# Agent attention with a two-layer feed-forward: the linear part's left-over rows on two row groups, a different last sum, and eight key slots

## What is computed

```python
def sm(a, b):
    s = scale * (a @ b.transpose(0, 2, 1))
    s = s - s.max(-1, keepdims=True)
    e = np.exp(s)
    return e / (e.sum(-1, keepdims=True) + 1e-09)
agent_v = sm(agents, k) @ v
x = (sm(q, agents) @ agent_v).reshape(B * N, C)
h = x @ w_in
g = np.maximum(h, 0.0) + alpha * np.minimum(h, 0.0)
out = g @ w_out
```

## Time and profile before

| | |
|---|---|
| median of 3 runs | 918.34 us (917.63 to 918.72) |
| profiled execution, its own time | 918.38 us |
| its span | 916.5 us |
| TensorE (PE) busy | 907.9 us, 99% |
| VectorE (DVE) busy | 626.0 us, 68% |
| ScalarE (ACT) busy | 514.8 us, 56% |
| GpSimd (POOL) busy | 108.4 us, 12% |
| mean DMA traffic | 72 GB/s, 298 and 336 GB/s in the first two fortieths |

### The profile page before, as it was taken

One profiled execution on the slowest core, in us unless ns is written; L12 is line 12 of the kernel. 1 busy time (PEld: TensorE's weight loads), 2 busy tenths in 40 slices (PEclk: granted clock), 3 DMA queues, 4 the chain that ended last, 5 costly groups with the idle time before them and its releaser, 6 DMA issues.

```text
span 916.5 us, 16103 instructions
## 1 busy us (share of the span) xinstructions
PE 907.9 (99%) x5662; PEld 488.7 (53%) x5662; DVE 626.0 (68%) x923; ACT 514.8 (56%) x695; POOL 108.4 (12%) x138
## 2 busy tenths in 40 slices
PE   9999999999999999999999999999999999999998
PEld 9865555555555565555444444444444444444443
DVE  4567667677777777677776666767676766767664
ACT  2445555555555555656565655555565656566554
POOL 6500010010010010010010101001010101010101
PEclk9999999999999999999999999999999999999999
DMA  8952222221232233121121111111111212111100
GB/s 298 336 164 87 60 72 88 60 82 54 73 96 97 72 92 100 38 57 35 38 58 34 43 52 40 54 38 56 37 57 37 57 36 59 34 49 44 33 29 22
DMA packets 67813, 65.75 MB, mean 72 GB/s; under 512 B 38528, under 2 KB 63424, under 8 KB 67520
## 3 DMA queue, kind: packets, MB, share of 16 engines
q1 hardware_dynamic: 67488, 65.19, 23.8%
q10 hardware_dynamic: 288, 0.06, 0.0%
HBM read 40.49 MB, written 12.78 MB: 58 GB/s over the span
## 4 chain that ended last, share of the span: by engine, by line
PE 95%; DMA 2%; issue 2%; DVE 1%; SPq 0%; ACT 0%; POOLq 0%
PE ps L599 56%; PE ps L582 18%; PE ps L589 7%; PE ps L563 3%; PE ps L609 2%; PE ps L772 2%; PE ps L766 1%; PE ps L519 1%; PE ps L441 1%; DMA kv_s<-kT 1%; DMA w_inT_s<-w_inT 1%; PE ps L544 1%; DVE r_lo L1181 0%; PE ps L465 0%; PE ps L472 0%
## 5 line engine op out<-in xcount | busy, mean ns | idle before, releaser
L1181 DVE SCALAR_TENSOR_TENSOR r_lo<-ps,r_hi 128x960 f16<-128x960 f32 x416 | 466.5, 1153 | 248.0 <-ACT r_hi L938 245.6
L938 ACT ACTIVATE r_hi<-ps 128x960 f16<-128x960 f32 x416 | 386.2, 967 | 173.9 <-PE ps L589 173.8
L599 PE MATMUL ps<-r_hi,w_hi 128*128 128x480 f16 x832 | 252.1, 369 | 0.5 <-DVE r_lo L1181 0.5
L599 PE MATMUL ps<-r_hi,w_lo 128*128 128x480 f16 x832 | 248.0, 366 | 0.0
L599 PE MATMUL ps<-r_lo,w_hi 128*128 128x480 f16 x832 | 240.8, 366 | 0.0
L582 PE MATMUL ps<-PT,M_a 128*128 128x480 f16 x832 | 203.2, 366 | 0.3 <-DVE r_lo L1181 0.3
L426 POOL TENSOR_TENSOR y<-y_relu,y_lin 128x480 f32<-128x480 f32 x52 | 62.3, 1199 | 616.0 <-ACT y_relu L1019 443.6
L599 PEld LDWEIGHTS ps<-r_hi,w_lo 128*128 128x128 f16 x832 | 91.2, 110 | 68.8
L582 PEld LDWEIGHTS ps<-PT,M_a 128*128 128x128 f16 x832 | 81.1, 99 | 86.3 <-DVE r_lo L1181 2.1
L599 PEld LDWEIGHTS ps<-r_lo,w_hi 128*128 128x128 f16 x832 | 85.4, 106 | 71.2
L599 PEld LDWEIGHTS ps<-r_hi,w_hi 128*128 128x128 f16 x832 | 73.2, 106 | 81.5 <-issue 38.8
(11 more groups left out here) (153 smaller groups left out, 515.5 us busy)
## 6 DMA issues: line engine op xcount, KB each, us to landing
q_s<-qT SPq DMA_DIRECT2D x52, 240.0 KB, 2.6
out<-y SPq DMA_DIRECT2D x52, 240.0 KB, 2.0
kv_s<-kT SPq DMA_DIRECT2D x23, 512.0 KB, 4.3
kv_s<-vP SPq DMA_DIRECT2D x12, 512.0 KB, 9.5
kv_s<-vS SPq DMA_DIRECT2D x8, 768.0 KB, 4.4
PR<-PT SPq DMA_DIRECT2D x156, 32.0 KB, 1.8
PT<-stack SPq DMA_TRANSPOSE x208, 2.3
w_lin<-w_out SPq DMA_DIRECT2D x1, 1024.0 KB, 8.5
```

The source lines that it names most:

```text
L599: mm = pe.matmul(ps[:, OUT, 0:CHUNK], w[:, 2 * p + u, :], r[:, s, u, :], start=(p == 0 and u == 0 and k == 0), stop=(p == PAIRS - 1 and u ...
L938: act.activation(r_hi[:, p % RING, :, :], ps[:, at:at + 2, 0:CHUNK], ACT.Relu).then_inc(hi_ready, 1)
L1181: dve.scalar_tensor_tensor(out=r_lo[:, p % RING, :, :], in0=ps[:, at:at + 2, 0:CHUNK], scalar=0.0, in1=r_hi[:, p % RING, :, :], op0=ALU.ma ...
```

## The change

- linear: L_a as two matmuls of 240 columns into banks 0 and 1; the 32 rows that L_b really has come later, behind rest_of_quad(3), as two matmuls of 240 columns, one on row group 0 (PT) and one on row group 1 (PR). L_b has 64 rows, the 32 twice, and GpSimd no longer clears it. mix_linear writes the 32 rows to partitions 0 to 31 and 32 to 63.
- ScalarE takes y_lin after relu_hi of pair 6 instead of before it, from two banks. SyncE's turn waits for lin_ready instead of h_ready.
- The last chunk has no y_relu and no sum on GpSimd: VectorE adds bank 6, scaled, and y_lin in two halves of 240 columns; SyncE stores the first, ScalarE's queue the second.
- Keys go through all 8 slots, w_out is loaded behind piece 6, the values' first load waits until piece 8 has been scored; the clearing of slots 4 to 7 to ones stands behind piece 8, the maximum of w_relu behind piece 9, and relu_max_row behind piece 12. 5 and 3 matmuls on ones instead of 6 and 4.

```diff
+HALF = CHUNK // 2
+KEY_SLOTS = 2 * RING
...
-        L_b = sb("L_b", [128, B, C], F16)
-        L_rh = sb("L_rh", [32, C], F16)
+        L_b = sb("L_b", [64, B, C], F16)
+        L_rh = sb("L_rh", [64, C], F16)
...
             def load_keys(m):
-                s = (m - 1) % RING
-                if m > RING:
+                s = (m - 1) % KEY_SLOTS
+                if m > KEY_SLOTS:
 
-                    sp.wait_ge(k_scored, m - RING + 1)
+                    sp.wait_ge(k_scored, m - KEY_SLOTS + 1)
...
             def load_values(m):
+                if m == 1:
+
+                    sp.wait_ge(k_scored, KEY_SLOTS + 1)
...
                 load_keys(m)
-                if m == 3:
+                if m == 6:
                     sp.dma_start(w_lin[:, :, :], w_out).then_inc(in_wo, 16)
...
-                    sp.wait_ge(h_ready, groups)
+                    sp.wait_ge(lin_ready, parts)
...
-                    sp.wait_ge(y_ready, n + 1)
-                    sp.dma_start(out[n], y[:, half, :]).then_inc(stored[half], 16)
+                    if there(n + 1):
+
+                        sp.wait_ge(y_ready, n + 1)
+                        sp.dma_start(out[n], y[:, half, :]).then_inc(stored[half], 16)
+                    else:
+
+                        sp.wait_ge(last_y, 1)
+                        sp.dma_start(out[n][:, 0:HALF], y[:, half, 0:HALF]).then_inc(stored[half], 16)
...
-            pool.memset(L_b[:, :, :], 0.0).then_inc(consts, 1)
...
-                    finish(n, half, i)
+                    if there(n + 1):
+                        finish(n, half, i)
...
             def mix_linear(b, bank):
                 pe.wait_ge(b_avl, b + 1)
-                pe.matmul(ps[0:32, bank, C:2 * C], av_l[:, b, 128:SEL], lin_w[:, :], start=True, stop=True,
-                          skip_group_check=True)
+                for g in (0, 32):
+                    pe.matmul(ps[g:g + 32, bank, C:2 * C], av_l[:, b, 128:SEL], lin_w[:, :], start=True, stop=True,
+                              skip_group_check=True)
...
             def linear(half, b):
-                for w, end in ((L_a, False), (L_b, True)):
-                    mm = pe.matmul(by_tile(ps[:, 2 * LIN_SLOT, 0:CHUNK]), w[:, b, :], tokens(PT, half), start=not end,
-                                   stop=end)
+                for h in range(2):
+                    pe.matmul(by_tile(ps[:, 2 * LIN_SLOT + h, 0:HALF]), L_a[:, b, :], tokens(PT, half)[:, 2 * h:2 * h + 2, :],
+                              start=True, stop=False)
+
+
+            def rest_of_linear(half, b):
+                for h, src in enumerate((PT, PR)):
+                    at = slice(32 * h, 32 * h + 32)
+                    mm = pe.matmul(by_tile(ps[:, 2 * LIN_SLOT + h, 0:HALF]), L_b[at, b, :],
+                                   tokens(src[at, :, :], half)[:, 2 * h:2 * h + 2, :], start=False, stop=True)
                 mm.then_inc(lin_ready, 1)
...
-            warm(6)
+            warm(5)
             pe.wait_ge(in_agents, 16)
             tail_scores(0, SMALL)
-            warm(4)
+            warm(3)
             for m in range(1, FULL + 1):
                 first_scores(m)
-                if m == FULL - 1:
-
-                    pe.wait_ge(consts, 5)
-                    relu_max_row()
+
+            pe.wait_ge(consts, 4)
+            relu_max_row()
...
                     rest_of_quad(3, half, b)
+                    rest_of_linear(half, b)
                     second_layer(4, half)
...
+                    relu_hi(g + 6, quad + 3, 6, False)
                     act.wait_ge(lin_ready, n + 1)
                     if not (isinstance(i, int) and i == 0):
 
                         act.wait_ge(y_ready, n - 1)
-                    act.activation(y_lin[:, half, :], ps[:, 2 * LIN_SLOT, 0:CHUNK], ACT.Copy,
+                    act.activation(y_lin[:, half, :].rearrange("p (h n) -> p h n", n=HALF),
+                                   ps[:, 2 * LIN_SLOT:2 * LIN_SLOT + 2, 0:HALF], ACT.Copy,
                                    scale=lin_unscale[:, b, :]).then_inc(lin_saved, 1)
-                    relu_hi(g + 6, quad + 3, 6, False)
...
+                    else:
+
+                        act.wait_ge(last_y, 2)
+                        act.dma_start(out[n][:, HALF:CHUNK], y[:, half, HALF:CHUNK]).then_inc(stored[1 - half], 16)
...
-                if m == 7:
+                if m == 9:
                     dve.wait_ge(relu_w_in, 1)
                     dve.tensor_reduce(w_col[:, 0:1], w_relu[:, :, :], AX.XY, ALU.max,
                                       apply_absolute_value=True).then_inc(relu_col, 1)
-                if m == FULL - 1:
-                    relu_max_top()
+                if m == KEY_SLOTS:
+
+                    for s in range(RING, KEY_SLOTS):
+                        dve.memset(kv_s[:, s, 0:4 * RUN + 1:RUN], 1.0).then_inc(ones_in, 1)
             key_max_column(0)
+            relu_max_top()
...
+                    else:
+
+                        dve.wait_ge(lin_saved, n + 1)
+                        dve.wait_ge(pair_done, g + PAIRS)
+
+                        dve.wait_ge(stored[half], 16 * i)
+                        for at in (slice(0, HALF), slice(HALF, CHUNK)):
+                            dve.scalar_tensor_tensor(out=y[:, half, at], in0=ps[:, OUT, at], scalar=out_unscale[:, b, :],
+                                                     in1=y_lin[:, half, at], op0=ALU.mult, op1=ALU.add).then_inc(last_y, 1)
```

More of the change, by code:

```diff
@@ L152, in build @@
         in_agents, in_acol, in_wo, in_wT = sem("in_agents"), sem("in_acol"), sem("in_wo"), sem("in_wT")
-        in_k = [sem(f"in_k{s}") for s in range(RING)]
+        in_k = [sem(f"in_k{s}") for s in range(KEY_SLOTS)]
         in_v = [sem(f"in_v{s}") for s in range(2 * RING)]
@@ L184, in build @@
         h_ready, hi_ready, lo_ready, pair_done = sem("h_ready"), sem("hi_ready"), sem("lo_ready"), sem("pair_done")
-        lin_ready, lin_saved, relu_saved, y_ready = (
-            sem(x) for x in ("lin_ready", "lin_saved", "relu_saved", "y_ready"))
+        lin_ready, lin_saved, relu_saved, y_ready, last_y = (
+            sem(x) for x in ("lin_ready", "lin_saved", "relu_saved", "y_ready", "last_y"))
         first_keys = turn_sign[:, 0:PIECE // 128, :].rearrange("p t k -> p (t k)")
@@ L293, in turn @@
             def turn(n, half, read=None):
-                groups = QUADS * n - QUADS
+                parts = n - 1
                 if not isinstance(n, int):
-                    groups = sp.compute_val(groups)
+                    parts = sp.compute_val(parts)
                 sp.wait_ge(stack_zero, 1)
                 if read is not None:
-                    sp.wait_ge(h_ready, groups)
+                    sp.wait_ge(lin_ready, parts)
                 sp.wait_ge(q_hi, n + 1)
@@ L349, in body @@
                         spread(n + 2, half)
-                    sp.wait_ge(y_ready, n + 1)
-                    sp.dma_start(out[n], y[:, half, :]).then_inc(stored[half], 16)
+                    if there(n + 1):
[4 more added lines that the diff above has]
+                        sp.dma_start(out[n][:, 0:HALF], y[:, half, 0:HALF]).then_inc(stored[half], 16)
             each_body(sp, body)
-            for half in range(2):
-                sp.wait_ge(stored[half], 16 * BODIES)
+            sp.wait_ge(stored[0], 16 * BODIES + 16)
+            sp.wait_ge(stored[1], 16 * BODIES)
         @block.gpsimd
@@ L392, in over_channels @@
                 return x[:, :].rearrange("p (t o) -> p t o", o=1).to_broadcast(by_feature)
-            pool.wait_ge(consts, 5)
+            pool.wait_ge(consts, 4)
             pool.tensor_tensor(turn_sign[:, :, :], ident[:, :].rearrange("p (o c) -> p o c", o=1).to_broadcast(by_feature),
@@ L455, in first_scores @@
             def first_scores(m):
-                s = (m - 1) % RING
-                pe.wait_ge(in_k[s], 16 * ((m - 1) // RING + 1))
+                s = (m - 1) % KEY_SLOTS
+                pe.wait_ge(in_k[s], 16 * ((m - 1) // KEY_SLOTS + 1))
                 if m > 2:
@@ L740, in body @@
                     if keys:
-                        pe.wait_ge(in_k[half], 16 * i + 16 * (FULL // RING + 1))
+                        pe.wait_ge(in_k[half], 16 * i + 16 * (FULL // KEY_SLOTS + 2))
                     if kind == VALUES:
@@ L914, in linear_high @@
                 act.activation(L_a[:, b, :], ps[:, LIN_BANK[b], 0:C], ACT.Copy)
-                act.activation(L_rh[:, :], ps[0:32, LIN_BANK[b], C:2 * C], ACT.Copy).then_inc(l_high, 1)
+                act.activation(L_rh[:, :], ps[0:64, LIN_BANK[b], C:2 * C], ACT.Copy).then_inc(l_high, 1)
             def weights_high():
@@ L1016, in body @@
                         relu_hi(g + 9, quad + 4, 1, False)
-                    act.wait_ge(pair_done, g + PAIRS)
-                    act.activation(y_relu[:, half, :], ps[:, OUT, 0:CHUNK], ACT.Copy,
-                                   scale=out_unscale[:, b, :]).then_inc(relu_saved, 1)
+                    if there(n + 1):
```

(12 more changed lines are left out.)

## The result

The changed kernel takes 909.63 us (median of 4 runs, 909.03 to 910.06) against 918.53 for the kernel before beside it: a ratio of 0.9904, with a 95% interval of 0.9887 to 0.9921. The profiled execution took 909.56 us with a span of 907.8. The forecast was 910.5 with a range of 909.0 to 915.6.

The account below looks back on a forecast made before the run. The prediction took TensorE's own list of matmuls to bound the kernel over the chunks. Its terms, -4.4 - 2.2 - 1.25 = -7.85 us from 918.38, gave 910.5 us, with a range of 909.0 to 915.6.

Parts of the forecast that it names:

- The linear part: TensorE's matmuls per chunk: -0.10 us in 48 chunks, +0.10 in chunk 0 and the last three, -4.4 us in all.
- the small rival: L_a's halves on TensorE are bound by their weight loads at 0.12 us each, +0.035 per chunk, 912.2 us; chance 0.06.
- The reload rival: L_b's weight loads wait for the quad to stream, 0.09 us exposed per chunk, +4.7, 915.2 us; chance 0.14.
- ScalarE's moved y_lin: y_lin (0.66 us) between relu_hi 6 and 7 delays later relus, but TensorE's covers hold, so it costs nothing.
- The cover of relu_lo 7: On VectorE, relu_lo 7 ends at 615.0 and TensorE needs it at about 616.0, 1.0 us later.
- The opening: Key pieces follow without waits, turn_weights at about 27.8 instead of 30.03; -2.2 us, bounds 0 to -2.6.
- That the clock might rise late: In the opening, less work on ones delays the higher clock, or VectorE's maxima end last; 911.6 to 912.7 us; chance 0.10.
- The end: After the last matmul VectorE's two PSUM reads take 0.74 us instead of 2.01, second store issued 1.25 earlier; -1.25 us.
- The slower rival: The two short matmuls share nothing and drain separately, 0.41 us per chunk; +11.7 in place of -4.4, 926.6 us; chance 0.03.

Follow-up runs that it names:

- the run on one row group: Changed kernel with both 32-row matmuls of the linear rest on row group 0 instead of groups 0 and 1; 915.03 us, ratio 0.9964 to the kernel before.
- the run away from the quad: Changed kernel with the two 32-row matmuls directly behind L_a's halves instead of behind the quad's four; 919.92 us, 1.0012 of the kernel before.

## Why the prediction was right

**The linear part, -4.4 us.** It came to 4.7 to 4.8. Each term stood: L_a's halves 0.20 against 0.207, the pair 0.10 against 0.10, 15.53 against 15.54 per chunk. The reason held too, not only the sum: the run on one row group shows that the groups share the array, and the run away from the quad that the switch was already paid. The 0.3 to 0.4 that were missing: a chunk is 0.107 shorter (15.640 to 15.533), not 0.10, over 48 chunks. L_a's halves save the 0.20 counted (0.405 before, 0.205 after), and the pair costs 0.095. Chunk 0 and the last three lost 0.1 each, as said (tiles(7) idle 0.35). That the halves are bound by their loads, the small rival at 0.12 each, is out: they are 0.10 each, and one full matmul in their place takes 0.203.

**The reload rival** is refuted twice, by the loads at 589.24 and by the run on one group. What persuaded me, the mixing in the earlier trace rows, is of column groups and fp32. That row groups behave like it came out true, but no row before the change said so: so far the choice was partly luck.

**ScalarE's moved y_lin.** Its cost of nothing held. The cover of relu_lo 7 was read as 1.0 and is 1.2. But the prediction didn't ask what the order guards against: the run with y_lin first shows that relu_lo 6 has no cover at all in that order.

**The opening, -2.2 us** measured -2.6 by the profile and 2.55 by the run with the old opening. Each wait went as said: no wait for a key piece, none for w_inT, and VectorE's chain of maxima ended 0.35 ahead of key_max_rows. From piece 2's start to turn_weights it was 22.18 us and is 20.06: 2.1, the forecast's 2.2 less the 0.1 that it gave to an earlier start. The other 0.5 lies ahead: piece 1 starts at 5.52, counted as 5.9, since the row couldn't say when it lands, and piece 2 at 7.38 instead of 7.86. In the profile this is in part luck: in the six others with this opening turn_weights came at 27.49 to 28.03, 2.0 to 2.5 earlier than before. That the clock might rise late was the right thing to fear: with the wait for piece 2 it moves this stretch by half a microsecond from one execution to another. The evidence against it, the clock of 1.00 in the earlier trace rows, could not have told, since the same view prints 1.00 in the run without matmuls on ones; what tells are the 30 records in 3 us.

**The end, -1.25 us** measured -1.35. The two reads of PSUM took 0.84 instead of 0.74 and began 0.10 behind the matmul, so the store was issued 1.05 to 1.1 earlier, not 1.25; two stores of half the size then ended about 0.3 sooner after their issue (2.2 instead of 2.5), which I had only in the bound.

**The slower rival** was right about a mechanism, the price of a change of shape, though for another place: it needed 0.25 us for the pair to decide, and the pair costs 0.31 where it stands alone.

## What to carry to other kernels

Small matmuls on row groups cost columns only when they follow others of the same shape; between full matmuls each visit costs about 0.2 us besides. So gather them behind a visit that is there already, and split them over groups and banks. And when a wait of the bounding engine is found, the same costly form can be free inside it: place by place, not kernel by kernel.

## What was not expected of the hardware

- A weight load for a row group began within 0.02 us of the start of a matmul on the same group and cost nothing (589.24, and 0.10 from half to half on one group). The sum counted on it, but no row before the change showed it.
- The granted clock first reads high at 4.2 to 4.4 us in three of the seven profiles with the same opening, with turn_weights at 27.44 to 27.68, and at 6.1 to 7.0 in the four others, with turn_weights at 27.83 to 28.03. What sets it among these no run here shows.
- Two stores of 120 KB on two queues ended the span 2.2 us after the later issue, one of 240 KB 2.5 after its own (the same in the run with the old end).
